# Copying the even cosine and sine tables to scratch DRAM in six parts, in a Fourier and two-layer network kernel

## The reference

```python
# x: (4, 3008, 256); both networks: 256 -> 2048 -> 256, over 12032 tokens
X = np.fft.fft(x, axis=1)
X = np.fft.fft(X, axis=2)
x = X.real.astype(np.float32).reshape(12032, 256)
r = np.maximum(x @ moe_w_in, 0.0)
x = (r * r) @ moe_w_out
h = x @ moe2_w_in
out = (h * np.cos(h)) @ moe2_w_out
```

## Time and profile before

| | |
|---|---|
| median of three runs | 1948.14 us |
| the profiled execution | 1947.55 us |
| its span, first to last instruction | 1945.4 us |
| granted TensorE clock, mean | 0.999 |
| PE busy | 1923.3 us (99%) |
| DVE busy | 1433.4 us (74%) |
| ACT busy | 1262.5 us (65%) |
| share of the chain that ended last | PE 96%, DVE 2%, DMA 2%, ACT 1% |
| PE waits for `gh` from DVE, whole run | 5.7 us |
| `scratch_t<-tables` | 2 DMAs of 4536 KB, median 17.8 us to landing |

### The profile page before, as it was taken

One profiled execution on the slowest core, in us unless ns is written; L12 is line 12 of the kernel. 1 busy time (PEld: TensorE's weight loads), 2 busy tenths in 40 slices (PEclk: granted clock), 3 DMA queues, 4 the chain that ended last, 5 costly groups with the idle time before them and its releaser, 6 DMA issues.

```text
span 1945.4 us, 21326 instructions
## 1 busy us (share of the span) xinstructions
PE 1923.3 (99%) x8452; PEld 1590.3 (82%) x8452; DVE 1433.4 (74%) x1665; ACT 1262.5 (65%) x1321; POOL 0.2 (0%) x4
## 2 busy tenths in 40 slices
PE   7999999999999999999999999999999999999999
PEld 5878888888888888888888888888888888888887
DVE  8968877876876877677787687676677777767665
ACT  6857756755765765676676576566567667567554
POOL 0000000000000000000000000000000000000000
PEclk9999999999999999999999999999999999999999
DMA  8731103113112211200111311210000000000000
GB/s 322 250 114 54 62 27 104 37 36 120 54 52 89 64 62 44 76 6 0 54 33 41 110 54 51 75 46 6 11 22 6 11 22 6 0 22 1 1 11 21
DMA packets 36835, 106.08 MB, mean 55 GB/s; under 512 B 4152, under 2 KB 14648, under 8 KB 36288
## 3 DMA queue, kind: packets, MB, share of 16 engines
q1 hardware_dynamic: 36224, 90.80, 13.8%
q10 hardware_dynamic: 512, 13.93, 2.0%
HBM read 86.18 MB, written 27.82 MB: 59 GB/s over the span
## 4 chain that ended last, share of the span: by engine, by line
PE 96%; DVE 2%; DMA 2%; ACT 1%; issue 0%; SPq 0%; ACTq 0%
PE ps L931 96%; DMA stage_a<-w2i 1%; DMA x<-x 1%; DVE gh L851 0%; DVE fold_all L733 0%; ACT tab_even L532 0%; DVE fold_all L738 0%; DVE weo L717 0%; DVE kbuf L886 0%; ACT gh L683 0%; DVE u L891 0%; ACT u L677 0%; ACT u L684 0%; DVE u L892 0%; SPq L347 0%
## 5 line engine op out<-in xcount | busy, mean ns | idle before, releaser
L931 PE MATMUL ps<-gh,wo 128*128 128x502 f32 x4608 | 1124.2, 393 | 5.7 <-DVE gh L851 5.7
L931 PEld LDWEIGHTS ps<-gh,wo 128*128 128x128 f32 x4608 | 871.6, 189 | 196.0 <-DVE gh L851 7.7
L931 PE MATMUL ps<-y,wi 128*128 128x502 f32 x2304 | 555.2, 390 | 0.0
L931 PEld LDWEIGHTS ps<-y,wi 128*128 128x128 f32 x2304 | 434.2, 189 | 88.2
L898 DVE TENSOR_TENSOR u<-kbuf,ps 128x1004 f32<-128x1004 int32 x192 | 230.5, 1201 | 347.2 <-ACT kbuf L692 347.1
L851 DVE TENSOR_TENSOR gh<-u,gh 128x1004 fp32r<-128x1004 f32 x384 | 459.9, 1198 | 3.8 <-ACT u L684 2.7
L692 ACT ACTIVATE kbuf<-ps 128x1004 int32<-128x1004 f32 x192 | 193.9, 1010 | 350.2 <-PE ps L931 349.2
L677 ACT ACTIVATE u<-u 128x1004 f32<-128x1004 f32 x192 | 200.8, 1046 | 165.4 <-DVE u L892 165.3
L931 PE MATMUL ps<-eo,weo 128*128 128x502 f32 x1152 | 292.5, 389 | 0.2 <-DVE eo L820 0.2
L931 PEld LDWEIGHTS ps<-eo,weo 128*128 128x128 f32 x1152 | 216.6, 188 | 46.2 <-DVE est L776 0.9
L704 ACT ACTIVATE u<-u 128x1004 f32<-128x1004 f32 x192 | 200.5, 1044 | 65.6 <-DVE u L898 65.6
(11 more groups left out here) (82 smaller groups left out, 325.7 us busy)
## 6 DMA issues: line engine op xcount, KB each, us to landing
ring<-scratch_t SPq DMA_DIRECT2D x72, 378.0 KB, 4.0
xin<-x SPq DMA_DIRECT2D x36, 512.0 KB, 3.3
out<-osb SPq DMA_DIRECT2D x23, 502.0 KB, 3.5
scratch_t<-tables ACTq DMA_DIRECT2D x2, 4536.0 KB, 17.8
raw<-scratch_eo SPq DMA_DIRECT2D x11, 502.0 KB, 5.2
scratch_eo<-est SPq DMA_DIRECT2D x14, 376.5 KB
stage_t<-tables SPq DMA_DIRECT2D x6, 756.0 KB, 17.3
tab_odd<-scratch_t ACTq DMA_DIRECT2D x2, 2268.0 KB, 11.7
```

What stands on the lines that cost most here:

```text
L931: op = pe.matmul(out_, a, b, start=start and i == 0, stop=stop and i == len(todo) - 1)
```

## The change

The one copy of the even table, issued in chunk 12 of tile 0, becomes six copies of 756 KB, one for each of the six parts, issued in chunks 8 to 13 of tile 0. Each is a copy of 128 rows of 6048 bytes; the copy before was one flat range, which the build lays out as 96 rows of 48384 bytes. SP waits for the sum of the six copies. The copy of the odd table is as it was.

```diff
+EVEN_COPIES = range(8, 8 + 2 * KT)
...
-        for odd in range(2):
-            sp.wait_ge(tab_st[odd], 16)
+        sp.wait_ge(tab_st[0], 16 * 2 * KT)
+        sp.wait_ge(tab_st[1], 16)
...
-        def copy_tables(odd):
-            act.dma_start(scratch_t[odd].rearrange("p t o h k -> (p t) (o h k)"),
-                          tables[odd].rearrange("p t o h k -> (p t) (o h k)")).then_inc(tab_st[odd], 16)
+        def copy_odd_tables():
+            act.dma_start(scratch_t[1].rearrange("p t o h k -> (p t) (o h k)"),
+                          tables[1].rearrange("p t o h k -> (p t) (o h k)")).then_inc(tab_st[1], 16)
+
+        def copy_even_tables(n):
+            act.dma_start(scratch_t[0, :, n], tables[0, :, n]).then_inc(tab_st[0], 16)
...
-        copy_tables(1)
+        copy_odd_tables()
...
-            if it.t == 0 and it.kind == "up" and it.index == 12:
-                copy_tables(0)
+            if it.t == 0 and it.kind == "up" and it.index in EVEN_COPIES:
+                copy_even_tables(EVEN_COPIES.index(it.index))
```

## The result

The changed kernel takes 1941.61 us (median of 7 runs, 1941.23 to 1943.06), the kernel before 1948.14 (7 runs, 1947.27 to 1949.85): a ratio of 0.9968, with a 95% interval of 0.9956 to 0.9979. It is faster by 6.5 us in the medians. The profiled executions are 1941.23 and 1947.55 us, 6.3 apart.

The account below looks back on a forecast made before the run. PE was taken to bound the kernel, held by a late load of weight part 14. 1947.55 less 4.49 (wait) and 1.66 (slow clock) gives 1941.4; with 0.59 for the median, 1942.0 us, range 1941.0 to 1945.5.

Parts of the forecast that it names:

- The wait of 4.49 us: PE idle from 105.04 to 109.53, before the down products of chunks 14 and 15; forecast to go entirely.
- part 14: Weight load on q1, issued at 86.50, 18.09 us beside the copy; forecast to land at 94.3, wanted at 96.7.
- Rival 3: A load completes only when what q10 had begun before is done; time stays at 1948; chance 0.06.
- Rival 1: Gain partly given back: loads of parts 11 to 13 late by 1 to 4 us, short PE waits; 1944.5; chance 0.13.
- The term of 1.66 us: Extra time of 24 down-product matmuls after PE's wait, 7.12 against 5.46 us, laid to the lower clock; forecast to go.
- the slow stretch: PE's 7.1 us after the wait, granted clock 0.76, partly at 1.2 GHz after PE had stood idle.
- p: Time of one pair, a 6 KB copy packet and a 2 KB load packet; taken as 0.44 us, range 0.32 to 0.53.
- The 0.28 and 0.16: Forecast us per packet: 0.28 for the copy's (an eighth of 2.26), 0.16 for a load's; together 0.44.
- The lower bound of the prediction, 0.32: Least pair time: 0.235 us for a streamed 6 KB row plus 0.086 for a 2 KB packet with nothing beside.
- Zero cost for six issues: On ACT, six copy issues in place of one were taken to add nothing, each 0.53 us hidden.
- the lead: ACT's sequencer runs some 2 us or more ahead of the engine, so issues of 0.53 to 1.73 us hide.
- Rival 2: Fixed charge per DRAM to DRAM packet, 0.57 rather than 0.28 us; PE loses 10.5 us, 1952.5, slower; chance 0.07.

Follow-up runs that it names:

- The first experiment: Against the kernel before: six copies of 6 KB rows in place of one copy, all issued in chunk 12; 1941.94 us, ratio 0.9969.

## Why the prediction was right

**The wait and its cause.** The forecast was 1942.0 us, the result 1941.61. The wait of 4.49 us is gone, and its cause is shown from both sides: the same moment with short packets has no wait, and behind a doubled flat copy part 14 landed at 109.6, after 8 long packets' time. Rival 3, a load that waits for what is ahead of it, would have 105 there, and in the run with every copy twice it would have parts 12 and 14 over 4 us later than they came. Rival 1 did not come either: PE has no wait between 60 and 125 us.

**The clock.** The term of 1.66 us was right in size: 7.12 became 5.54 us. The reason was put loosely. Not every wait brings the slow stretch: in the profiled runs waits of 1.72 and 0.42 us did not, 4.49 did.

**The pair.** The mechanism held, its size was too high. I took p = 0.44 us; the changed kernel has 0.23 for the copy's packet and 0.245 x 6 x 16 / 277 = 0.085 for the load's, 0.32 together, and parts 10 and 11 landed 2.6 us apart, 8 x 0.33. The 0.28 and 0.16 were read from the copy of before, where a long packet took 2.26 us and not 1.8 as with little beside it; why they slow each other was not tried. The lower bound of the prediction, 0.32, was the right value. Part 10 was forecast for 80.2 and landed at 80.1, which is partly luck: q10 came free at 77.3 and not at 76.7, and the smaller p made up for it. Part 11 was forecast for 83.7 and landed at 82.7, part 12 for 87.3 and landed at 85.0, part 13 for 90.8 and landed at 86.1. Part 14, forecast for 94.3, landed at 94.1, which is no merit of the rule: it was issued at 86.45, a load with nothing beside it takes 3.0 us, eight packets of the copy add 8 x 0.23 = 1.9, and it took 7.7. Of the rest of some 3 us, about 1.4 is a late start: its first packet came at 88.8, 2.4 us after the issue, where the same load alone began within 1.0 us (flat copy in chunk 15). Strict turns would have let it in behind one packet of the copy. This may be what held parts 12 and 13 with the rows of 1512 bytes; why it happens, and the other 1.4 us, stays open.

**The issues.** Zero cost for six issues was right, at 0.50 us each and spread over six chunks. The first experiment shows how near the other outcome is: six in a row are too many for the lead.

**Rival 2.** There is no charge worth naming for a DRAM to DRAM packet: 0.23 us for 6048 bytes (26 GB/s) against 1.8 us for 48384 (27 GB/s). The Trainium skill's advice of DMAs of 1 MiB and more (DMA: Bandwidth & Descriptors, section Bandwidth), from which I had worked out 0.59 us for each packet, rests there on figures for loads to SBUF that GpSimd issues, and does not apply to DMAs of 756 KB that stand one behind the other on a queue.

**What I did not foresee.** I took the cut into short packets for the cause of the gain. Either half of the change does it all: short packets at the old moment, or long ones in six pieces some 4 us apart. What they have in common is that no load or store stands beside six or more long packets in a row. The copy in chunk 15 was my own miss of the same kind: I listed the loads beside the new place and left out a store.

## What to carry to other kernels

When two DMA queues are at work, a small transfer was held here for about as many of the other queue's packets as it has itself on each DMA engine, and at times some us longer; so look at how long the other's packets are (its megabytes over its packets), not only at its bytes. A background copy that is a flat range is built with the longest packets; give it the rows of its tile, or issue it in small parts, and list every DMA, stores too, that falls beside it. What such a wait costs is read on the engine that bounds the kernel, with the clock after it.

## What the runs showed of the hardware

- In the profiled runs TensorE's clock fell to the lower level only with the long waits. Granted clock 1.00 after 1.72 and 0.42 us and after 1.55 us, 0.76 over the 7.1 us after a wait of 4.49, and after 9.42 us the down product of 12 matmuls took 5.29 us where 2.73 is usual. The stretch of it, with PEclk 0.52:

```profile
114.50:119.85 5.35, 5.29 (x12) 3.82 (x12) 0.01 (x1) 0.00 (x0) 0.00 (x0) 0.52 0.85 277
```

- A flat DRAM range of 4.5 MB moved in packets of 48384 bytes. One of them took 1.8 us with little beside it and 2.26 us in the copy of before.
- ACT issued a DMA that stands behind two of its own instructions before these ran, at 85.99 with the ReLU behind it at 89.02; six issues in a row used that up and held the engine 0.87 us.
